# Swapping which engine copies which half of an expert's results, splitting the first chunk on two engines, and adding row sums with a reduction

## The chip, the cores and the metric

The kernel runs on one core of one Trainium2 chip. The core has a matrix engine (TensorE, in profiles PE, with its weight loads as PEld), a vector engine (VectorE, DVE), a scalar engine (ScalarE, ACT), a general engine (GpSimd, POOL) and a queue that issues transfers (SyncE, SP). Each works through its own list of instructions in order; they wait for each other through semaphores. The metric is the device time of one launch in microseconds. Three runs of the kernel before took 813.53, 816.81 and 817.45 us; the median is 816.81.

## The reference

Three layers follow each other: an attention in which a query sees only the keys of its own cluster, a mixture of eight experts with one expert for each token, and a layer with a rational activation. All is float32. Cut to what matters:

```python
# attention: 2 batches x 8 heads, 768 tokens, width 64, 16 clusters per head
mask = argmax(q_n @ c_n.T)[:, None] == argmax(k_n @ c_n.T)[None, :]
scores = where(mask, scale * q @ k.T, -1e9)
attn = exp(scores - rowmax)
attn = attn / (attn.sum(-1) + 1e-09)
x = attn @ v                                   # 1536 tokens x 512
# experts: 8, hidden width 1024, one expert per token
e, gate = argmax and its softmax weight of (xn @ en.T / tau)
x = gate * (maximum(x @ w1[e], 0) @ w2[e])
# last layer: hidden width 2048
h = x @ w_in
g = (a0 + a1*h + a2*h^2 + a3*h^3) / (1 + |b0|*|h| + |b1|*h^2 + 1e-6)
out = g @ w_out
```

## The kernel before, in words

Every float32 product is made of three products of rounded parts: a value is split into a high part (rounded to the format fp32r) and a low part (the value less the high part), and TensorE multiplies high by high, high by low and low by high (lines 489 to 491). So each operand needs a rounding copy and a subtraction, and these are spread over the engines.

**Attention.** Sixteen heads follow each other; a loop handles two heads a pass. A head has six row blocks (`i` = 0 to 5). For each block TensorE makes the scores, VectorE takes the row maximum (`rowmax`, NM, L953), ScalarE takes the exponential and its row sum (PR and SM, L624), TensorE transposes (L401), ScalarE makes the high part PTH (L651) and VectorE the low part PTL (L1040). TensorE's transposes of block `i` wait for the exponential of that block and for the two PTL halves of the block before. Beside this VectorE finds the clusters of the next head (`one_hots`, L963 to L971), and twice a head it turns three row sums into factors (`inverse_sums`, RS, L980 and L982): once behind block 4, and once behind block 1 of the next head. GpSimd splits the next head's operands (A, B) and values (VS, L855 and L857), and in heads 3 to 10 also one piece of the first expert's weights (`high_piece`, L825).

**Experts.** Tokens are sorted by expert and handled in chunks of 256 tokens; here each expert has one chunk, so there are eight. An expert has eight weight pieces of 128x1024 values: GpSimd rounds them (w_high, L825), VectorE subtracts (w_low, L1024). A chunk has a first product (four banks, rectified by ScalarE into HH, L734, and by VectorE into HL, L1171) and a second product into two banks, 6 and then 7. ScalarE copies bank 6 into YT rows 0 and 1 once the first half of the second product is done, while TensorE works on the second half; VectorE copies bank 7 into YT rows 2 and 3 at the end.

**The junction.** The last layer needs YT split into XH and XL. For the first chunk this is done by halves (`cut_first`): ScalarE rounds, VectorE subtracts. In between, ScalarE also rounds pieces 0 to 3 of w_out (L801). VectorE then makes w_low of pieces 4 to 7 of w_in. TensorE starts on the first half of three hidden pairs (`first_products`) when the first XL is there, and on the rest when the second is.

**The last layer.** Six chunks of eight hidden pairs. For a pair, ScalarE and VectorE evaluate the rational function in turns (VectorE lines 1220, 1222, 1224, 1231, 1233, 1235), ScalarE rounds it into HH (L759), GpSimd subtracts into HL (L901), and TensorE's second product of that pair, three pairs behind, waits for HL. In the first chunk VectorE makes w_low of one piece of w_out within each pair, between L1224 and L1231. GpSimd has to finish its rounding of w_out pieces 4 to 7 before its first HL.

The order on every engine is written out by hand; nothing is scheduled by a program.

Of the kernel before, what the change touches and what calls it, by code (L numbers as in the profile page):

```python
# [52 lines left out]
def program(nc, q, k, v, cent, emb, tau, w1, w2, w_in, w_out, coef_a, coef_b, cst, tokid, out, dbg=None):  # L53
# [4 lines left out]
    with ExitStack() as ctx:  # L58
# [64 lines left out]
        SM = esb("SM", [P, 2, JT])  # L123
# [49 lines left out]
        w_high, w_high_act, w_low = sem("w_high"), sem("w_high_act"), sem("w_low")  # L173
# [5 lines left out]
        yh_done, yl_done, g3_done, g4_done = (sem(n) for n in ("yh_done", "yl_done", "g3_done", "g4_done"))  # L179
# [31 lines left out]
        def _(sp):  # L211
# [44 lines left out]
            sp.wait_ge(pool_ready, 6)  # L256
# [64 lines left out]
        def _(pe):  # L321
# [268 lines left out]
        def _(act):  # L590
# [27 lines left out]
            def exp(g, par, i):  # L618
                n = JT * g + i
                act.wait_ge(max_done, n + 1)  # L620
                if needed(2 * n - 2):
# [3 lines left out]
                                     accum_out=SM[:, par, i:i + 1]).then_inc(exp_done, 1)  # L625
# [100 lines left out]
            with act.Fori(0, E // 2) as ep:  # L726
                for par in range(2):
                    lo, hi, off = bounds(act, 2 * ep + par)
                    with act.Fori(lo, hi) as i:
                        for fp in range(4):  # L730
                            if fp == 2:
# [7 lines left out]
                        act.wait_ge(y_ps, 2 * i + 1)  # L739
                        nc.scalar.activation(YT[:, 0:2, bass.ds(column(off, lo, i), CH)],  # L740
                                             PS[:, 6, :].rearrange("p (a t) -> p a t", a=2), ACT.Copy).then_inc(y_act, 1)
# [53 lines left out]
            total, = bounds(act, E - 1, (1,))  # L795
            act.wait_ge(y_act, total + 1)
            act.wait_ge(xl_done, total + 1)
# [16 lines left out]
        def _(pool):  # L814
# [5 lines left out]
            nc.gpsimd.memset(OH[:, :, :], 0.0).then_inc(pool_ready, 1)  # L820
            nc.gpsimd.memset(zeros[:, :], 0.0).then_inc(pool_ready, 1)
# [46 lines left out]
            pool.wait_ge(pool_ready, 6)  # L868
# [53 lines left out]
        def _(dve):  # L922
# [53 lines left out]
            def inverse_sums(g, par, grp):  # L976
# [3 lines left out]
                nc.vector.tensor_scalar(RS[:, :], SM[:, par, GT * grp:GT * (grp + 1)], 1e-9, None, ALU.add).then_inc(rs_done, 1)  # L980
# [233 lines left out]
            def layer_chunk(c, cpar, start=False, end=False):  # L1214
                for j in range(PAIRS):
# [9 lines left out]
                    if start:  # L1225
                        low_piece(E + 1, 1, j)
# [52 lines left out]
```

## Time and profile before

| what | value |
|---|---|
| median of three runs | 816.81 us |
| the profiled execution's own time | 815.08 us |
| its span, first to last instruction | 813.3 us |
| TensorE busy | 747.3 us, 92% of the span |
| VectorE busy | 607.1 us, 75% |
| ScalarE busy | 468.9 us, 58% |
| GpSimd busy | 350.1 us, 43% |
| mean granted TensorE clock | 0.969 of full speed |
| attention | about 0 to 300 us |
| routing of the tokens, TensorE nearly idle | about 300 to 329 us |
| experts | about 329 to 530 us |
| last layer | about 531 to 806 us |

The profile describes one execution. A row of the timeline has the start and the duration of one instruction (or of several alike, with their count), the engine, the line, the operation and, in brackets, how long the engine had been idle before and which instruction released it. The granted clock is the share of TensorE's full speed that the chip allowed in a stretch.

### The profile page before, as it was taken

The numbers are of one execution on the slowest core, as the hardware profiler recorded it, in microseconds if no ns is written. First come the engines' busy times: TensorE is split into PE (matmuls) and PEld (weight loads), VectorE is DVE, ScalarE is ACT, GpSimd is POOL, SyncE is SP. The second block draws the span as 40 slices with busy tenths as digits, with TensorE's granted clock in tenths as the row PEclk, the third lists the DMA queues.
The fourth block names the chain that finished last, engine by engine and source line by source line (L and its number), as shares of the span: only waits on it lengthen the run. The fifth ranks groups of instructions, "written<-read, shape, count | busy, mean of one in ns | idle before, by whom it ended". The sixth has DMA issues, their size and how long they took to land.

```text
span 813.3 us, 15460 instructions
## 1 busy us (share of the span) xinstructions
PE 747.3 (92%) x5289; PEld 695.2 (85%) x5290; DVE 607.1 (75%) x977; ACT 468.9 (58%) x884; POOL 350.1 (43%) x330
## 2 busy tenths in 40 slices
PE   7899999999999840699999999979999999999996
PEld 4799899998999730699999999979999999999995
DVE  4788888888888863356766666799987877877773
ACT  4677777778777850212222112457777767777672
POOL 3666757766566108204443344532232222322232
PEclk9999999999999985699999999999999999999999
DMA  9311112111110037224666444830000000000000
GB/s 266 85 32 31 39 29 48 29 29 39 29 58 1 0 107 278 63 97 175 225 235 232 158 170 169 286 104 1 1 27 1 26 3 1 26 0 26 0 26 27
DMA packets 67907, 64.66 MB, mean 80 GB/s; under 512 B 30872, under 2 KB 53528, under 8 KB 67872
## 3 DMA queue, kind: packets, MB, share of 16 engines
q1 hardware_dynamic: 65024, 57.29, 22.0%
q0 software_dynamic: 1920, 6.70, 2.1%
q8 instruction: 19, 0.31, 0.2%
q10 hardware_dynamic: 928, 0.23, 0.1%
q14 instruction: 16, 0.13, 0.0%
HBM read 56.92 MB, written 7.29 MB: 79 GB/s over the span
## 4 chain that ended last, share of the span: by engine, by line
PE 49%; issue 24%; DVE 13%; POOL 9%; ACT 3%; DMA 1%; POOLq 0%; DVEq 0%; ACTq 0%
PE PS L489 8%; PE PS L490 8%; PE PS L491 8%; PE PS L401 6%; POOL HL L901 6%; PE PS L375 3%; PE PS L376 3%; PE PS L360 3%; PE PS L361 3%; PE PS L342 3%; DVE NM L953 2%; DVE PTL L1040 2%; POOL xs_dram L892 2%; POOL out L910 1%; PE PS L384 1%
## 5 line engine op out<-in xcount | busy, mean ns | idle before, releaser
L489 PE MATMUL PS<-XH,w_high 128*128 128x256 f32 x640 | 182.9, 286 | 5.6 <-DVE XL L1163 2.5
L490 PE MATMUL PS<-XL,w_high 128*128 128x256 f32 x640 | 182.5, 285 | 0.0
L491 PE MATMUL PS<-XH,w_low 128*128 128x256 f32 x640 | 182.4, 285 | 0.0
L825 POOL TENSOR_SCALAR w_high<-w_raw 128x1024 fp32r<-128x1024 f32 x76 | 96.6, 1290 | 132.9 <-DMA w_raw<-in_moe_w 107.3
L901 POOL TENSOR_TENSOR HL<-U,HH 128x512 fp32r<-128x512 f32 x48 | 62.6, 1303 | 185.8 <-ACT HH L759 185.8
L489 PEld LDWEIGHTS PS<-XH,w_high 128*128 128x128 f32 x640 | 124.2, 194 | 8.6 <-issue 4.9
L490 PEld LDWEIGHTS PS<-XL,w_high 128*128 128x128 f32 x640 | 124.1, 194 | 1.8
L1040 DVE TENSOR_TENSOR PTL<-PS,PTH 128x384 fp32r<-128x384 f32 x192 | 97.9, 551 | 36.4 <-ACT PTH L651 36.3
L491 PEld LDWEIGHTS PS<-XH,w_low 128*128 128x128 f32 x640 | 124.0, 194 | 0.0
L1024 DVE TENSOR_TENSOR w_low<-w_raw,w_high 128x1024 fp32r<-128x1024 f32 x80 | 111.5, 1423 | 9.3 <-issue 9.2
L651 ACT ACTIVATE PTH<-PS 128x384 fp32r<-128x384 f32 x192 | 84.7, 489 | 45.3 <-PE PS L401 44.9
L953 DVE TENSOR_REDUCE NM<-PS 128x1 f32<-128x768 f32 x96 | 90.9, 948 | 2.6 <-PE PS L361 2.6
L401 PE MATMUL PS<-consts,PR 128*128 128x128 f32 x576 | 82.8, 278 | 9.8 <-ACT PR L624 5.1
L624 ACT ACTIVATE PR<-PS,NM 128x768 f32<-128x768 f32 x96 | 86.9, 905 | 5.5 <-DVE NM L953 5.3
L401 PEld LDWEIGHTS PS<-consts,PR 128*128 128x128 f32 x576 | 65.7, 143 | 19.2 <-DVE PTL L1040 7.9
L734 ACT ACTIVATE HH<-PS 128x512 fp32r<-128x512 f32 x32 | 19.1, 598 | 108.9 <-PE PS L491 108.9
L489 PE MATMUL PS<-w_high,HH 128*128 128x512 f32 x192 | 76.1, 396 | 2.8 <-POOL HL L901 2.8
L490 PE MATMUL PS<-w_low,HH 128*128 128x512 f32 x192 | 75.8, 395 | 0.0
L491 PE MATMUL PS<-w_high,HL 128*128 128x512 f32 x192 | 75.2, 392 | 0.0
L360 PE MATMUL PS<-B,A 128*128 128x512 f32 x192 | 73.3, 382 | 0.8 <-POOL A L866 0.8
L489 PE MATMUL PS<-HH,w_high 128*128 128x256 f32 x256 | 73.2, 286 | 0.0
L490 PE MATMUL PS<-HL,w_high 128*128 128x256 f32 x256 | 72.5, 283 | 0.0
(174 smaller groups left out, 1702.2 us busy)
## 6 DMA issues: line engine op xcount, KB each, us to landing
w_raw<-in_moe_w SPq DMA_DIRECT2D x64, 512.0 KB, 8.2
xs<-xs_dram SPq DMA_DIRECT2D x9, 578.0 KB, 7.7
w_raw<-in_moe_w_in SPq DMA_DIRECT2D x8, 512.0 KB, 8.2
w_raw<-in_moe_w_out SPq DMA_DIRECT2D x8, 512.0 KB, 6.3
QK<-in_q SPq DMA_DIRECT2D x16, 192.0 KB, 3.1
V<-in_v SPq DMA_DIRECT2D x16, 192.0 KB, 2.3
QK<-in_k SPq DMA_DIRECT2D x15, 192.0 KB, 3.2
xs_dram<-zeros SPq DMA_DIRECT2D x1, 578.0 KB, 3.3
```

The source lines that it names most:

```text
L360: nc.tensor.matmul(o[:, lo:hi], A1[par][:, cols], B1[par][:, lo:hi], start=True, stop=False)
L401: last = nc.tensor.transpose(pt_bank[hf][:, j * P:(j + 1) * P], PR[i % 2][:, c:c + P], ident)
L489: nc.tensor.matmul(o, wh, xh, start=first, stop=False)
L490: nc.tensor.matmul(o, wh, xl, start=False, stop=False)
L491: return nc.tensor.matmul(o, wl, xh, start=False, stop=last)
L624: nc.scalar.activation(PR[i % 2][:, :], s_bank(i % 2), ACT.Exp, bias=NM[:, par, i:i + 1], accum_out=SM[:, par, i:i + 1]).then_inc(exp_done, 1)
L651: nc.scalar.activation(PTH[grp][:, 3 * hf:3 * hf + 3, at:at + P], pt_bank[hf].rearrange("p (a q) -> p a q", a=3), ACT.Copy).then_inc(pth_d ...
L825: return nc.gpsimd.tensor_scalar(HIGH[par][:, p, :], RAW[par][:, p, :], 1.0, 0.0, ALU.mult, ALU.add)
L901: nc.gpsimd.tensor_tensor(HL[:, g:g + 2, :].rearrange("p a t -> p (a t)"), U[j % 2][:, :], HH[:, g:g + 2, :].rearrange("p a t -> p (a t)") ...
L953: nc.vector.tensor_reduce(NM[:, par, i:i + 1], s_bank(i % 2), AX.X, ALU.max, negate=True).then_inc(max_done, 1)
L1024: nc.vector.tensor_tensor(LOW[par][:, p, :], RAW[par][:, p, :], HIGH[par][:, p, :].bitcast(F32), ALU.subtract).then_inc(w_low, 1)
L1040: nc.vector.tensor_tensor(PTL[i // GT][:, 3 * hf:3 * hf + 3, at:at + P], pt_bank[hf].rearrange("p (a q) -> p a q", a=3), PTH[i // GT][:, 3 ...
```

## The change

Four edits.

1. **Row sums.** SM gets a second column next to each sum, filled once with 1e-9 by GpSimd. In `inverse_sums` VectorE adds each pair with `tensor_reduce`, where it added the constant 1e-9 with `tensor_scalar`.
2. **Expert results.** VectorE copies bank 6 (rows 0 and 1, after the first half of the second product); ScalarE copies bank 7 (rows 2 and 3, at the end).
3. **First chunk.** Rows 0 and 1 are rounded by VectorE itself (a `tensor_scalar`) and subtracted there; rows 2 and 3 are rounded by ScalarE. ScalarE no longer rounds pieces of w_out: GpSimd rounds all eight.
4. **First pair.** In the last layer's first pair, VectorE makes the low part of w_out piece 0 at the end of the pair and not in its middle.

```diff
-        SM = esb("SM", [P, 2, JT])
+        SM = esb("SM", [P, 2, JT, 2])
...
+            nc.gpsimd.memset(SM[:, :, :, 1:2], 1e-9).then_inc(pool_ready, 1)
...
-                nc.vector.tensor_scalar(RS[:, :], SM[:, par, GT * grp:GT * (grp + 1)], 1e-9, None, ALU.add).then_inc(rs_done, 1)
+                nc.vector.tensor_reduce(RS[:, :], SM[:, par, GT * grp:GT * (grp + 1), :], AX.X, ALU.add).then_inc(rs_done, 1)
...
-                        act.wait_ge(y_ps, 2 * i + 1)
-                        nc.scalar.activation(YT[:, 0:2, ...], PS[:, 6, :]..., ACT.Copy).then_inc(y_act, 1)
+                        act.wait_ge(y_ps, 2 * i + 2)
+                        nc.scalar.activation(YT[:, 2:4, ...], PS[:, 7, :]..., ACT.Copy).then_inc(y_act, 1)
...
-            act.wait_ge(y_act, total + 1)
             act.wait_ge(xl_done, total + 1)
-            cut_first(0)
-            for p in range(4):
-                act.wait_ge(raw_in[1][p // 2], 32 * (E // 2) + 32)
-                nc.scalar.activation(HIGH[1][:, p, :], RAW[1][:, p, :], ACT.Copy).then_inc(w_high_act, 1)
-            act.wait_ge(y_dve, total + 1)
+            act.wait_ge(y_act, total + 1)
             cut_first(1)
...
-                for p in range(4 if w == E + 1 else 0, 8):
+                for p in range(8):
                     high_piece(w, w % 2, p).then_inc(w_high, 1)
...
-                dve.wait_ge(y_ps, 2 * i + 2)
-                nc.vector.tensor_copy(YT[:, 2:4, ...], PS[:, 7, :]...).then_inc(y_dve, 1)
+                dve.wait_ge(y_ps, 2 * i + 1)
+                nc.vector.tensor_copy(YT[:, 0:2, ...], PS[:, 6, :]...).then_inc(y_dve, 1)
...
+                if n == 0:
+                    dve.wait_ge(y_dve, total + 1)
+                    dve.wait_ge(xl_done, total + 1)
+                    nc.vector.tensor_scalar(XH[0][:, 0:2, :], YT[:, 0:2, 0:CH], 1.0, 0.0, ALU.mult, ALU.add).then_inc(yh_done, 1)
...
-                    if start:
+                    if start and j:
                         low_piece(E + 1, 1, j)
...
+                    if start and j == 0:
+                        low_piece(E + 1, 1, 0)
```

The first place is on VectorE, in the loop over heads, behind block 1: before

```order
94 L969 TENSOR_REDUCE AM<-AEQ 128x12 [waits arg_step]
96 L971 TENSOR_TENSOR OH<-AEQ,AM 128x6x2x16 [waits arg_step]
98 L953 TENSOR_REDUCE NM<-PS 128x1 [waits s_done]
100 L980 TENSOR_SCALAR RS<-SM 128x3 [waits exp_done]
102 L982 RECIPROCAL RS<-RS 128x3 [waits rs_done]
```

and now:

```order
94 L965 TENSOR_REDUCE AM<-AEQ 128x12 [waits arg_step]
96 L967 TENSOR_TENSOR OH<-AEQ,AM 128x6x2x16 [waits arg_step]
98 L949 TENSOR_REDUCE NM<-PS 128x1 [waits s_done]
100 L976 TENSOR_REDUCE RS<-SM 128x3 [waits exp_done]
102 L978 RECIPROCAL RS<-RS 128x3 [waits rs_done]
```

Nothing moved here; one instruction has another kind, and keeps its wait.

The second place is on VectorE at the junction, from the split of the first chunk to the end of the last layer's first pair. Before:

```order
407 L1203 TENSOR_TENSOR XL<-YT,XH 128x512 [waits yh_done] x2
408 L1024 TENSOR_TENSOR w_low<-w_raw,w_high 128x1024 [waits w_high] x4
409 L1220 TENSOR_TENSOR PS<-PS,AH 128x512 [waits t_done]
410 L1222 TENSOR_TENSOR U<-U,PS 128x512
411 L1224 SCALAR_TENSOR_TENSOR U<-U,minus_a,PS 128x512 [waits v_done]
412 L1024 TENSOR_TENSOR w_low<-w_raw,w_high 128x1024 [waits w_high_act]
413 L1231 SCALAR_TENSOR_TENSOR PS<-PS,R 128x512 [waits r0_done]
414 L1233 SCALAR_TENSOR_TENSOR R<-PS,R 128x512 [waits n_done]
415 L1235 SCALAR_TENSOR_TENSOR U<-U,minus_a,R 128x512 [waits r_done]
416 L1220 TENSOR_TENSOR PS<-PS,AH 128x512 [waits t_done]
```

and now:

```order
409 L1199 TENSOR_SCALAR XH<-YT 128x512 [waits xl_done,y_dve]
410 L1203 TENSOR_TENSOR XL<-YT,XH 128x512 [waits yh_done]
411 L1203 TENSOR_TENSOR XL<-YT,XH 128x512 [waits yh_act]
412 L1017 TENSOR_TENSOR w_low<-w_raw,w_high 128x1024 [waits w_high] x4
413 L1220 TENSOR_TENSOR PS<-PS,AH 128x512 [waits t_done]
414 L1222 TENSOR_TENSOR U<-U,PS 128x512
415 L1224 SCALAR_TENSOR_TENSOR U<-U,minus_a,PS 128x512 [waits v_done]
416 L1231 SCALAR_TENSOR_TENSOR PS<-PS,R 128x512 [waits r0_done]
417 L1233 SCALAR_TENSOR_TENSOR R<-PS,R 128x512 [waits n_done]
418 L1235 SCALAR_TENSOR_TENSOR U<-U,minus_a,R 128x512 [waits r_done]
419 L1017 TENSOR_TENSOR w_low<-w_raw,w_high 128x1024 [waits w_high]
420 L1220 TENSOR_TENSOR PS<-PS,AH 128x512 [waits t_done]
```

VectorE gets one rounding more, and the low part of the first w_out piece stands behind the first pair's last step.

The third place is on GpSimd, from the end of w_in's pieces to the first HL. Before:

```order
210 L825 TENSOR_SCALAR w_high<-w_raw 128x1024 [waits raw_in0_2] x2
211 L825 TENSOR_SCALAR w_high<-w_raw 128x1024 [waits raw_in0_3] x2
212 L825 TENSOR_SCALAR w_high<-w_raw 128x1024 [waits raw_in1_2] x2
213 L825 TENSOR_SCALAR w_high<-w_raw 128x1024 [waits raw_in1_3] x2
214 L901 TENSOR_TENSOR HL<-U,HH 128x512 [waits gh_done] x8
```

and now:

```order
211 L821 TENSOR_SCALAR w_high<-w_raw 128x1024 [waits raw_in0_2] x2
212 L821 TENSOR_SCALAR w_high<-w_raw 128x1024 [waits raw_in0_3] x2
213 L821 TENSOR_SCALAR w_high<-w_raw 128x1024 [waits raw_in1_0] x2
214 L821 TENSOR_SCALAR w_high<-w_raw 128x1024 [waits raw_in1_1] x2
215 L821 TENSOR_SCALAR w_high<-w_raw 128x1024 [waits raw_in1_2] x2
216 L821 TENSOR_SCALAR w_high<-w_raw 128x1024 [waits raw_in1_3] x2
217 L897 TENSOR_TENSOR HL<-U,HH 128x512 [waits gh_done] x8
```

Four roundings stand ahead of the four that were there.

## Rows read from the trace of the kernel before

**Rows 1.** Busy time by stage, loop over heads: engines' busy us (instructions), clock, DMA.
```profile
60.00:250.00 190.00, 186.05 (x1359) 173.25 (x1357) 163.86 (x329) 147.46 (x327) 127.18 (x133) 1.00 0.14 36
```

**Rows 2.** TensorE's waits: for whom, us in total, times, longest.
```profile
PE PS L401 <- DVE PTL L1040: 4.7, 13, 0.4
```

**Rows 3.** Line 980 over the span: ns least/median/most.
```profile
L980 DVE TENSOR_SCALAR RS<-SM x32: 155/159/772, 38.2 to 292.9; 128x3 f32<-128x3 f32 x32
```

**Rows 4.** Timeline of VectorE, blocks 0 and 1: start, us, instruction.
```profile
63.40 0.36 DVE L971 TENSOR_TENSOR OH<-AEQ,AM 128x192 bf16<-128x192 f32 x1
63.68 0.95 DVE L953 TENSOR_REDUCE NM<-PS 128x1 f32<-128x768 f32 x1
64.55 0.70 DVE L980 TENSOR_SCALAR RS<-SM 128x3 f32<-128x3 f32 x1
...
65.40 1.02 DVE L1040 TENSOR_TENSOR PTL<-PS,PTH 128x384 fp32r<-128x384 f32 x2
...
266.38 0.70 DVE L980 TENSOR_SCALAR RS<-SM 128x3 f32<-128x3 f32 x1
```

**Rows 5.** Timeline of GpSimd, the same stretch.
```profile
63.40 0.73 POOL L855 TENSOR_SCALAR VS<-V 128x384 fp32r<-128x384 f32 x1 [1.02 <-PE PS L376]
64.21 1.01 POOL L857 TENSOR_TENSOR VS<-V,VS 128x384 fp32r<-128x384 f32 x1
```

**Rows 6.** Timeline of ScalarE, the same: end of block 2's exponential.
```profile
65.55 0.19 ACT L624 ACTIVATION_READ_ACCUMULATOR PR<-PS,NM 128x1 f32 x1
```

**Rows 7.** Timeline of TensorE, the transposes of blocks 2 and 3.
```profile
66.02 1.01 PE L401 MATMUL PS<-consts,PR 128*128 128x128 f32 x6 [0.37 <-DVE PTL L1040]
66.79 0.48 PE L360 MATMUL PS<-B,A 128*128 128x512 f32 x1
...
68.96 0.81 PE L401 MATMUL PS<-consts,PR 128*128 128x128 f32 x6
69.53 0.48 PE L360 MATMUL PS<-B,A 128*128 128x512 f32 x1
```

**Rows 8.** Timeline of VectorE and GpSimd, first head.
```profile
27.19 0.35 DVE L969 TENSOR_REDUCE AM<-AEQ 128x12 f32<-128x192 f32 x1
27.58 1.48 DVE L971 TENSOR_TENSOR OH<-AEQ,AM 128x192 bf16<-128x192 f32 x1
...
27.02 1.82 POOL L845 TENSOR_TENSOR B<-T,B 64x768 fp32r<-64x768 f32 x1
```

**Rows 9.** Timeline of VectorE and ScalarE, between experts 6 and 7.
```profile
505.94 0.69 DVE L1179 COPY YT<-PS 128x512 f32 x1 [3.26 <-PE PS L491]
...
508.56 0.60 ACT L734 ACTIVATE HH<-PS 128x512 fp32r<-128x512 f32 x1 [7.84 <-PE PS L491]
```

**Rows 10.** Timeline of VectorE, junction.
```profile
530.44 1.47 DVE L1203 TENSOR_TENSOR XL<-YT,XH 128x512 fp32r<-128x512 f32 x2
...
537.76 0.70 DVE L1220 TENSOR_TENSOR PS<-PS,AH 128x512 f32<-128x512 f32 x1 [0.46 <-ACT PS L785]
...
539.75 1.22 DVE L1024 TENSOR_TENSOR w_low<-w_raw,w_high 128x1024 fp32r<-128x1024 f32 x1
...
542.34 1.09 DVE L1235 SCALAR_TENSOR_TENSOR U<-U,minus_a,R 128x512 f32<-128x512 f32 x1
```

**Rows 11.** Timeline of GpSimd, junction.
```profile
534.72 3.50 POOL L825 TENSOR_SCALAR w_high<-w_raw 128x1024 fp32r<-128x1024 f32 x2 [10.35 <-DMA w_raw<-in_moe_w_out]
539.82 3.07 POOL L825 TENSOR_SCALAR w_high<-w_raw 128x1024 fp32r<-128x1024 f32 x2 [1.60 <-DMA w_raw<-in_moe_w_out]
544.17 1.28 POOL L901 TENSOR_TENSOR HL<-U,HH 128x512 fp32r<-128x512 f32 x1 [1.28 <-ACT HH L759]
```

**Rows 12.** Timeline of TensorE, junction.
```profile
531.18 0.39 PE L489 MATMUL PS<-XH,w_high 128*128 128x256 f32 x1 [1.64 <-DVE XL L1203]
...
545.50 0.51 PE L489 MATMUL PS<-w_high,HH 128*128 128x512 f32 x1 [2.56 <-POOL HL L901]
```

**Rows 13.** Busy time and granted clock behind the junction.
```profile
546.00:552.00 6.00, 6.00 (x30) 5.20 (x29) 5.89 (x9) 4.52 (x8) 1.28 (x1) 0.72 0.01 3
```

More of the change, by code:

```diff
@@ L172, in program @@
         raw_in = [[sem(f"raw_in{n}_{i}") for i in range(4)] for n in range(2)]
-        w_high, w_high_act, w_low = sem("w_high"), sem("w_high_act"), sem("w_low")
+        w_high, w_low = sem("w_high"), sem("w_low")
         tau_in, xs_scaled = sem("tau_in"), sem("xs_scaled")
@@ L178, in program @@
         hh_done, hl_done, y_ps, y_act, y_dve = (sem(n) for n in ("hh_done", "hl_done", "y_ps", "y_act", "y_dve"))
-        yh_done, yl_done, g3_done, g4_done = (sem(n) for n in ("yh_done", "yl_done", "g3_done", "g4_done"))
+        yh_done, yh_act, yl_done, g3_done, g4_done = (sem(n) for n in ("yh_done", "yh_act", "yl_done", "g3_done", "g4_done"))
         ah_done, u_done, t_done, root_done, r0_done = (sem(n) for n in ("ah_done", "u_done", "t_done", "root_done", "r0_done"))
@@ L795, in _ @@
             total, = bounds(act, E - 1, (1,))
+            act.wait_ge(xl_done, total + 1)
             act.wait_ge(y_act, total + 1)
-            act.wait_ge(xl_done, total + 1)
-            cut_first(0)
-            for p in range(4):
-                act.wait_ge(raw_in[1][p // 2], 32 * (E // 2) + 32)
-                nc.scalar.activation(HIGH[1][:, p, :], RAW[1][:, p, :], ACT.Copy).then_inc(w_high_act, 1)
-            act.wait_ge(y_dve, total + 1)
             cut_first(1)
@@ L1019, in low_piece @@
             def low_piece(w, par, p):
-                if isinstance(w, int) and w == E + 1:
-                    dve.wait_ge((w_high_act, w_high)[p // 4], (p + 1, 8 * w + p - 3)[p // 4])
-                else:
-                    dve.wait_ge(w_high, 8 * w + p + 1)
+                dve.wait_ge(w_high, 8 * w + p + 1)
                 nc.vector.tensor_tensor(LOW[par][:, p, :], RAW[par][:, p, :], HIGH[par][:, p, :].bitcast(F32), ALU.subtract).then_inc(w_low, 1)
@@ L1177, in chunk @@
                         low_piece(e + 1, 1 - par, p)
-                dve.wait_ge(y_ps, 2 * i + 2)
-                nc.vector.tensor_copy(YT[:, 2:4, bass.ds(column(off, lo, i), CH)],
-                                      PS[:, 7, :].rearrange("p (a t) -> p a t", a=2)).then_inc(y_dve, 1)
+                dve.wait_ge(y_ps, 2 * i + 1)
+                nc.vector.tensor_copy(YT[:, 0:2, bass.ds(column(off, lo, i), CH)],
+                                      PS[:, 6, :].rearrange("p (a t) -> p a t", a=2)).then_inc(y_dve, 1)
             dve.drain().then_inc(y_dve, 1)
@@ L1200, in cut_first @@
             def cut_first(n):
-                dve.wait_ge(yh_done, n + 1)
+                if n == 0:
+                    total, = bounds(dve, E - 1, (1,))
+                    dve.wait_ge(y_dve, total + 1)
+                    dve.wait_ge(xl_done, total + 1)
+                    nc.vector.tensor_scalar(XH[0][:, 0:2, :], YT[:, 0:2, 0:CH], 1.0, 0.0, ALU.mult, ALU.add).then_inc(yh_done, 1)
+                    dve.wait_ge(yh_done, 1)
+                else:
+                    dve.wait_ge(yh_act, 1)
                 nc.vector.tensor_tensor(XL[0][:, 2 * n:2 * n + 2, :], YT[:, 2 * n:2 * n + 2, 0:CH], XH[0][:, 2 * n:2 * n + 2, :].bitcast(F32),
```

18 lines of the change are left out of this document (9 added, 9 removed).

## The prediction

> **What bounds the kernel now.** I read the busy time by stage first. In the loop over heads TensorE is busy for 186.05 of 190 us at full clock [rows 1]: it is the bound, and only its gaps can be won. TensorE's list of waits says whose they are: 13 times it waits for VectorE's PTL, 4.7 us in total, never over 0.4 us [rows 2]. These are one wait per head. I followed it back on VectorE's timeline, and there stands a suspicious row: the addition of a constant to three numbers takes 0.70 us [rows 4]. Over the span that instruction takes 155 ns at least, 159 ns in the median and 772 ns at most [rows 3]; on the timeline it is long 14 times, each time behind block 1, the last at 266.38 us [rows 4], and short behind block 4.
>
> Why it is long is seen on GpSimd: its VS subtraction runs from 64.21 to 65.22 us [rows 5], and the small addition, which started at 64.55, ends at 65.25 [rows 4]. VectorE did not compute for 0.70 us; it was held until GpSimd's instruction was over, and the PTL that TensorE needs starts at 65.40 behind it.
>
> At the junction of experts and last layer TensorE waits 1.64 us for the first XL and 2.56 us for the first HL [rows 12], and behind that the granted clock is 0.72 for 6 us [rows 13].
>
> **The change part by part.** *Row sums.* 14 held instructions lose their hold if the reduction is not held. In the first head a `tensor_reduce` from SBUF took 0.35 us beside a running GpSimd subtraction (27.02 to 28.84 us), while the `tensor_tensor` with two SBUF inputs right behind it took 1.48 us and ended when GpSimd had (29.06) [rows 8]. So reductions pass. The new one reads 6 elements for a partition where that one read 192; it costs between 0 and 0.35 us. I take 0.16, the median of the old one [rows 3], since both are tiny. VectorE then gains 0.70 - 0.16 = 0.54 us a head.
>
> The Trainium skill ("SBUF — State Buffer", practical consequences of the port rules) says that `copy`, `cast` and `tensor_scalar` can take the port pair shared with GpSimd, that it is an exclusive lock, and that `tensor_reduce` on trn2 never contends. The held `tensor_scalar` and the reduction that passed agree with it.
>
> How much of 0.54 reaches TensorE? PTL would start at 64.86, and its first half, 0.51 us (half of 1.02), be there at 65.4, the second at 65.9 [rows 4]. TensorE is free at 66.02 - 0.37 = 65.65 [rows 7]. But its transposes of block 2 also need block 2's exponential, and ScalarE ends that at 65.55 + 0.19 = 65.74 [rows 6]; it hangs on the row maximum at 63.68, ahead of the saved time. So TensorE starts at about 65.80 and not 66.02: 0.22 us. Next, the transposes of block 2 take 66.79 - 66.02 = 0.77 us to the next product, where those of block 3 take 69.53 - 68.96 = 0.57 us [rows 7]; the second three wait for the second PTL half. That one is now in time: 0.20 us more. Together 0.42 us a head. What is late next is the exponential, by 0.15 us. Heads: 13, by the waits [rows 2]; at the fourteenth, in the last pair of heads, ScalarE has extra squares to do and holds TensorE, so I count nothing. 13 x 0.42 = 5.5 us. The lower end is 13 x 0.22 = 2.9, the upper 13 x (0.37 + 0.20) = 7.4 us.
>
> *The fill of SM with 1e-9* is one small fill on GpSimd at the start. VectorE and GpSimd wait for it, but long before they have inputs: nothing. If that cover were gone it would be some 0.1 to 0.2 us once.
>
> *The swap of the result copies.* Both are off TensorE's path. In the middle of the second product VectorE now has the 0.7 us copy, and at the end ScalarE. ScalarE's last copy ends near 506.6, where VectorE's does now, and its first rectification comes at 508.56, after 7.84 us of idleness [rows 9]: 1.9 us are left for the loop's register loads. If these took longer, HH and HL would be late, but TensorE needs HL only after all four banks of the first product. Nothing, eight times. Behind ScalarE's wait only that rectification is queued.
>
> *The first chunk's split.* XH and XL of rows 0 and 1 can be made while TensorE works on the second half of the last expert, where before the XL waited behind VectorE's final copy. If nothing holds VectorE, the wait of 1.64 us [rows 12] goes. But VectorE's next steps do not come sooner: the second XL still ends at about 531.9 [rows 10] and the four w_low pieces behind it near 537.3, so the first pair's chain starts at 537.3 and not 537.76, 0.46 us earlier [rows 10]. TensorE's early start is given back at its next wait, the first HL.
>
> *GpSimd's four extra roundings.* GpSimd is idle for 10.35 us before 534.72 [rows 11], and 4 pieces at 1.5 us (half of 3.07) take 6 us. They fit into the gap, if their data is there, which ScalarE used without a wait.
>
> *The moved w_low piece* takes 1.22 us out of the first pair's chain [rows 10], about 1.1 without the overlap at its start. The first HH could come 0.46 + 1.1 = 1.6 us earlier. GpSimd however ends its last pieces at 542.89 and makes HL from 544.17 [rows 11]: at most 1.28 us can be won. Against that, w_low now stands where HL wants to start, and the last step L1235 took 1.09 us with GpSimd active [rows 10]. If HL is held for the rest of one w_low, some 0.8 us go. And the second pair's chain hardly starts earlier, as VectorE's total work is the same. The clock will drop again behind the wait: nothing won there.
>
> Junction in all: 1.3 us won at best; 0.5 lost at worst short of a rival below, if VectorE's new rounding and both XL are each held by one of GpSimd's new pieces. I take 0.5 us won, near the middle. VectorE's rounding of 128x512 has no row; it lies between 0.16 [rows 3] and 0.69, the copy of that size [rows 9], and I use 0.5; it is hidden unless held.
>
> By the same page of the Trainium skill this step speaks against the change: the new rounding is a `tensor_scalar` and the subtractions have two SBUF inputs, so each can be blocked by GpSimd's four new pieces. By that rule alone the junction would win 0.4 us and not 1.3.
>
> **Sum.** 5.5 + 0.5 = 6.0 us. The profiled execution took 815.08 us, so 809.1 on its own terms. It lies 1.73 us below the median of 816.81; the mean of the three runs is 815.9. I predict 815.9 - 6.0 = 810.
>
> **Rivals.** *Saved but given back:* the exponential, or GpSimd's masks of the next head, sets the pace as soon as PTL is earlier, and the second wait stays. Then 2.9 us and nothing at the junction: 813. For it: only 0.15 us lie between the old bound and the next. Against it: blocks 3 to 5 have idle engines before them.
>
> *No effect:* the reduction is held too, or the long row has another cause. Only the junction's 0.5 remains: 815.4. Against it stand rows 8, for it only that they show one case.
>
> *A new hold, slower:* in each head VectorE's OH starts at 63.40, in the same moment as GpSimd's VS rounding [rows 4, 5], and it has two SBUF inputs. When it comes second it is held, as in the first head: 1.48 instead of 0.36 us, 1.12 more [rows 4, 8]. The row maximum, the exponential and TensorE's transposes would follow: start at 65.80 + 1.12 = 66.92 and not 66.02, less 0.20 for the second half: 0.7 us a head, 13 x 0.7 = 9.1 us, so about 824 with the junction at -0.5. It decides once OH comes after GpSimd's start. Against it: both starts hang on TensorE's work of that block, which the change doesn't shift against them, and in the heads of the loop OH was never held.
>
> *More:* the full 7.4 us in attention, 1.3 at the junction, and the clock, 6 us at 0.72, so 6 x 0.28 = 1.7 us, stays up [rows 13]: 815.9 - 10.4 = 805.5. Against it: the first HL stays a wait of over 2 us.
>
> **How the numbers follow.** A difference of 0.5% of the median, 4.1 us, is about what a measurement can tell from no change; faster means under 812.7, slower over 820.9. Forecast 0.70, own range 806.5 to 813.5, of which 0.60 is faster and 0.10 same. Given back 0.11: 0.04 faster, 0.07 same. No effect 0.06, same 0.05 and slower 0.01. Slower rival 0.05. More 0.08, all faster. Faster 0.72, same 0.22, slower 0.06. The range runs from 804.5 to 814.5.
>
> **What would show it.** Right: all 32 row sums at about 0.16 us; TensorE's waits for PTL gone or replaced by about 0.15 us for ScalarE's PR; one head (201.83 us for the 12 from 64.55 to 266.38, so 16.82 us) shorter by 0.42 us; at the junction the first TensorE wait under 1.1 us, a second one of over 2 us, and the clock low behind it. Wrong: a row sum of 0.7 us; OH at over 1 us; a head as long as before; TensorE waiting in the experts for YT, HH or HL.

## The result, and the profile after

| kernel | median of 7 runs | from - to | ratio to before |
|---|---|---|---|
| before | 816.08 us | 813.53 - 817.45 | |
| changed | 812.65 us | 810.43 - 813.88 | 0.9959, 95% interval 0.9941 to 0.9977 |

The change gains 3.4 us (1.9 to 4.8 by the interval), where 6.0 were forecast. The profiled execution of the changed kernel took 812.02 us, its span is 810.1 us and its mean clock 0.968; before it was 815.08, 813.3 and 0.969. Line numbers have shifted: RS is L976 (was L980), PTL L1033 (L1040), NM L949 (L953), HL L897 (L901), w_low L1017 (L1024), w_high L821 (L825).

First the row sums, over the whole span (it answers to [rows 3]):

```profile
L976 DVE TENSOR_REDUCE RS<-SM x32: 146/148/158, 38.3 to 289.3; 128x3 f32<-128x6 f32 x32
```

The longest of 32 now takes 158 ns; the hold is gone. Fourteen of them still start while GpSimd's VS subtraction runs, and take 0.15 us each; in the kernel before the 14 in that place were the long ones. TensorE's waits for the PTL halves, against [rows 2], and the loop over heads, against [rows 1]:

```profile
PE PS L401 <- ACT PR L624: 5.4, 8, 1.4
PE PS L401 <- DVE PTL L1033: 2.5, 12, 0.2
```

```profile
60.00:250.00 190.00, 187.47 (x1378) 176.15 (x1378) 161.16 (x336) 149.88 (x334) 129.10 (x136) 1.00 0.14 36
```

The waits are shorter but still there, 0.2 us each. TensorE is busy for 1.4 us more of the same 190. The timeline of the stretch of [rows 4 to 7], VectorE and GpSimd first, then ScalarE, then TensorE:

```profile
63.12 0.36 DVE L967 TENSOR_TENSOR OH<-AEQ,AM 128x192 bf16<-128x192 f32 x1
63.40 0.95 DVE L949 TENSOR_REDUCE NM<-PS 128x1 f32<-128x768 f32 x1
64.27 0.15 DVE L976 TENSOR_REDUCE RS<-SM 128x3 f32<-128x6 f32 x1
64.45 0.18 DVE L978 RECIPROCAL RS<-RS 128x3 f32<-128x3 f32 x1
64.57 1.02 DVE L1033 TENSOR_TENSOR PTL<-PS,PTH 128x384 fp32r<-128x384 f32 x2
```

```profile
63.12 0.73 POOL L851 TENSOR_SCALAR VS<-V 128x384 fp32r<-128x384 f32 x1 [1.00 <-PE PS L376]
63.93 1.00 POOL L853 TENSOR_TENSOR VS<-V,VS 128x384 fp32r<-128x384 f32 x1
```

```profile
65.27 0.19 ACT L624 ACTIVATION_READ_ACCUMULATOR PR<-PS,NM 128x1 f32 x1
```

```profile
65.60 0.87 PE L401 MATMUL PS<-consts,PR 128*128 128x128 f32 x6 [0.22 <-DVE PTL L1033]
66.22 0.48 PE L360 MATMUL PS<-B,A 128*128 128x512 f32 x1
```

The reduction starts inside GpSimd's subtraction (63.93 to 64.93) and ends inside it. PTL starts 1.17 us after NM's start and not 1.72. OH, which the slower rival feared for, still begins together with GpSimd's VS and takes 0.36 us. TensorE's gap went from 0.37 to 0.22 us, and the stretch from the transposes to the next product from 0.77 to 0.62. A head, by this row and the one of the same place eleven heads later, takes (247.55 - 65.60) / 11 = 16.54 us, where it took 16.82:

```profile
247.55 0.87 PE L401 MATMUL PS<-consts,PR 128*128 128x128 f32 x6 [0.21 <-DVE PTL L1033]
```

At the junction, VectorE (answers to [rows 10]), GpSimd [rows 11] and TensorE [rows 12]:

```profile
523.75 0.68 DVE L1172 COPY YT<-PS 128x512 f32 x1
524.46 0.56 DVE L1199 TENSOR_SCALAR XH<-YT 128x512 fp32r<-128x512 f32 x1
525.05 1.40 DVE L1203 TENSOR_TENSOR XL<-YT,XH 128x512 fp32r<-128x512 f32 x1
527.57 0.69 DVE L1203 TENSOR_TENSOR XL<-YT,XH 128x512 fp32r<-128x512 f32 x1 [1.11 <-ACT XH L752]
528.18 4.62 DVE L1017 TENSOR_TENSOR w_low<-w_raw,w_high 128x1024 fp32r<-128x1024 f32 x4
533.09 0.70 DVE L1220 TENSOR_TENSOR PS<-PS,AH 128x512 f32<-128x512 f32 x1 [0.29 <-ACT PS L785]
```

```profile
534.97 2.06 POOL L821 TENSOR_SCALAR w_high<-w_raw 128x1024 fp32r<-128x1024 f32 x2 [0.23 <-DMA w_raw<-in_moe_w_out]
538.31 1.51 POOL L897 TENSOR_TENSOR HL<-U,HH 128x512 fp32r<-128x512 f32 x1 [1.29 <-ACT HH L759]
```

```profile
526.51 0.39 PE L489 MATMUL PS<-XH,w_high 128*128 128x256 f32 x1 [0.58 <-DVE XL L1203]
...
539.88 0.50 PE L489 MATMUL PS<-w_high,HH 128*128 128x512 f32 x1 [1.60 <-POOL HL L897]
...
582.37 0.39 PE L491 MATMUL PS<-w_high,HL 128*128 128x512 f32 x1
...
587.63 0.47 PE L489 MATMUL PS<-w_high,HH 128*128 128x512 f32 x1 [2.00 <-ACT OUT L766]
```

The wait for the first XL fell from 1.64 to 0.58 us and the wait for the first HL from 2.56 to 1.60. The last row is new: TensorE wants to start on the second chunk's second product, whose banks still hold the first chunk's results, and waits 2.00 us until ScalarE has copied them (OUT, L766, at 586.91). The row ahead of it is the first chunk's last matmul into those banks: they were complete about 4 us before the copy began. No such wait was listed before. The granted clock moved with the waits: behind the first HL, against [rows 13], it is now 1.00, and the 0.72 stands behind the OUT wait:

```profile
540.00:546.00 6.00, 5.78 (x36) 5.07 (x36) 5.90 (x9) 4.49 (x9) 1.29 (x1) 1.00 0.01 3
...
586.00:592.00 6.00, 4.37 (x12) 3.50 (x13) 5.81 (x11) 5.21 (x9) 2.39 (x2) 0.72 0.01 3
```

### The profile page after: what moved, and what is told of

It is laid out like the page before. It is cut to its first block, busy times and chain, and to the rows that moved or that the text cites. A ratio compares the mean times of both kernels' runs of the same rounds, so it can differ in the third digit from the quotient of the medians.

```text
span 810.1 us, 15464 instructions
## 1 busy us (share of the span) xinstructions
PE 745.9 (92%) x5289; PEld 695.7 (86%) x5290; DVE 596.8 (74%) x978; ACT 463.4 (57%) x879; POOL 354.6 (44%) x335
## 4 chain that ended last, share of the span: by engine, by line
PE 47%; issue 25%; DVE 13%; POOL 9%; ACT 3%; DMA 1%; DVEq 0%; POOLq 0%; ACTq 0%
PE PS L489 8%; PE PS L491 7%; PE PS L490 7%; PE PS L401 6%; POOL HL L897 6%; PE PS L375 3%; PE PS L376 3%; PE PS L360 3%; PE PS L361 3%; PE PS L342 3%; DVE NM L949 2%; DVE PTL L1033 2%; DVE w_low L1017 2%; POOL xs_dram L888 2%; POOL out L906 1%
## 5 line engine op out<-in xcount | busy, mean ns | idle before, releaser
L821 POOL TENSOR_SCALAR w_high<-w_raw 128x1024 fp32r<-128x1024 f32 x80 | 100.6, 1277 | 126.6 <-DMA w_raw<-in_moe_w 107.2
L897 POOL TENSOR_TENSOR HL<-U,HH 128x512 fp32r<-128x512 f32 x48 | 62.7, 1307 | 188.4 <-ACT HH L759 188.4
L1033 DVE TENSOR_TENSOR PTL<-PS,PTH 128x384 fp32r<-128x384 f32 x192 | 98.0, 552 | 40.1 <-ACT PTH L651 40.0
L1017 DVE TENSOR_TENSOR w_low<-w_raw,w_high 128x1024 fp32r<-128x1024 f32 x80 | 108.6, 1387 | 0.9 <-issue 0.9
L949 DVE TENSOR_REDUCE NM<-PS 128x1 f32<-128x768 f32 x96 | 90.9, 948 | 2.6 <-PE PS L361 2.6
L401 PE MATMUL PS<-consts,PR 128*128 128x128 f32 x576 | 81.0, 277 | 8.0 <-ACT PR L624 5.4
L491 PE MATMUL PS<-HH,w_low 128*128 128x256 f32 x256 | 72.5, 283 | 0.0
```

Of the source, the lines that this page charges most:

```text
L401: last = nc.tensor.transpose(pt_bank[hf][:, j * P:(j + 1) * P], PR[i % 2][:, c:c + P], ident)
L491: return nc.tensor.matmul(o, wl, xh, start=False, stop=last)
L821: return nc.gpsimd.tensor_scalar(HIGH[par][:, p, :], RAW[par][:, p, :], 1.0, 0.0, ALU.mult, ALU.add)
L897: nc.gpsimd.tensor_tensor(HL[:, g:g + 2, :].rearrange("p a t -> p (a t)"), U[j % 2][:, :], HH[:, g:g + 2, :].rearrange("p a t -> p (a t)") ...
L949: nc.vector.tensor_reduce(NM[:, par, i:i + 1], s_bank(i % 2), AX.X, ALU.max, negate=True).then_inc(max_done, 1)
L1017: nc.vector.tensor_tensor(LOW[par][:, p, :], RAW[par][:, p, :], HIGH[par][:, p, :].bitcast(F32), ALU.subtract).then_inc(w_low, 1)
```

## How the segments are compared

Runs of one kernel spread over some 3 to 4 us, as much as the gain. Much of that goes with the granted clock: of the 40 runs of the kernel before that stood beside the experiments, the eight with a mean clock of 0.964 took 815.8 to 818.0 us, the six with 0.970 to 0.972 took 813.4 to 815.4. The profiles show where part of that lies: block 2 of the fourth head starts at 63.38 us in E9's profile and at 65.67 in E10's, though their attention is the same. So I compare segments of TensorE's timeline: the first transposes of the experts (L485), the first product with XH, the first with HL, the end of the span. One point of ScalarE's is added, the start of its first copy of OUT, since it will be needed. Each ratio further down is against runs of the kernel before that were taken with that experiment: their medians are 816.35 us for E1 to E4, 815.46 for E5 to E8 and 815.82 for E9 and E10.

| kernel | experts start | first XL [wait] | first HL [wait] | end | start to first XL | first XL to end | first XL to OUT copy |
|---|---|---|---|---|---|---|---|
| before | 329.10 | 531.18 [1.64] | 545.50 [2.56] | 813.3 | 202.1 | 282.1 | 60.45 |
| changed | 325.40 | 526.51 [0.58] | 539.88 [1.60] | 810.1 | 201.1 | 283.6 | 60.40 |
| E1 | 326.28 | 528.40 [1.64] | 542.96 [2.77] | 810.7 | 202.1 | 282.3 | 60.69 |
| E2 | 329.84 | 529.85 [0.59] | 543.26 [1.62] | 811.9 | 200.0 | 282.1 | 60.45 |
| E3 | 329.48 | 530.13 [0.59] | 543.52 [1.61] | 812.2 | 200.7 | 282.1 | 60.43 |
| E4 | 323.54 | 524.14 [0.58] | 537.54 [1.63] | 806.2 | 200.6 | 282.1 | 60.47 |
| E5 | 325.97 | 525.97 [0.60] | 540.58 [2.83] | 808.4 | 200.0 | 282.4 | 60.77 |
| E6 | 325.57 | 527.58 [1.64] | 541.28 [1.92] | 810.0 | 202.0 | 282.4 | 60.74 |
| E7 | 327.50 | 528.73 [0.60] | 541.97 [1.47] | 810.5 | 201.2 | 281.8 | 59.84 |
| E8 | 325.86 | 526.90 [0.67] | 540.15 [1.47] | 807.6 | 201.0 | 280.7 | 59.05 |
| E9 | 324.38 | 525.62 [0.60] | 538.89 [1.50] | 806.2 | 201.2 | 280.6 | 59.03 |
| E10 | 324.94 | 527.34 [1.64] | 541.38 [2.27] | 807.9 | 202.4 | 280.6 | 58.94 |

## Which edit brings the gain: E1 and E2

E1 is the kernel before with edit 1 alone (and the column of 1e-9 that it needs):

```diff
-                nc.vector.tensor_scalar(RS[:, :], SM[:, par, GT * grp:GT * (grp + 1)], 1e-9, None, ALU.add).then_inc(rs_done, 1)
+                nc.vector.tensor_reduce(RS[:, :], SM[:, par, GT * grp:GT * (grp + 1), :], AX.X, ALU.add).then_inc(rs_done, 1)
```

> The kernel before with the row sums alone changed (pairs added by the reduction). Theory: the attention gives all that the row sums can, 13 heads at about 0.28 us, so the experts' first transposes start at about 325.4 us and the whole is about 3.6 us shorter than before; the junction is as before (waits of 1.64 and 2.56 us, low clock behind the second). Rival: the shorter attention is given back or enlarged at the junction; then the difference to before is under 2 or over 5 us.

E2 is the changed kernel with the same edit the other way round, so with edits 2 to 4 alone.

> The changed kernel with the row sums as before. Theory: attention as before (transposes at about 329.1 us); the junction wins some 1.9 us at the first HL, but VectorE cannot follow, TensorE waits about 2 us for ScalarE's OUT copy in the second chunk and the clock drops behind it, so the whole is within 0.5 us of before. Rival: the three other edits have a value of their own, then it is 1.5 us or more below before; or they cost, then it is above.

Measured: E1 812.70 us (6 runs), ratio 0.995 (0.993 to 0.997), E2 815.70 us (12 runs), ratio 0.9996 (0.998 to 1.0011), beside 816.35 for the kernel before. The row sums alone bring all that can be measured; edits 2 to 4 alone bring, by E2's interval, at most 0.2% of 816, or 1.6 us. E2's row sums have their long form back, and TensorE's waits for PTL with them:

```profile
L975 DVE TENSOR_SCALAR RS<-SM x32: 150/159/774, 38.7 to 293.5; 128x3 f32<-128x3 f32 x32
```

```profile
PE PS L401 <- DVE PTL L1032: 4.2, 12, 0.4
```

## Why the old row sum was long: E3

E3 is the changed kernel with the same column of 1e-9, but added by an operation with two SBUF inputs:

```diff
-                nc.vector.tensor_reduce(RS[:, :], SM[:, par, GT * grp:GT * (grp + 1), :], AX.X, ALU.add)
+                nc.vector.tensor_tensor(RS[:, :], SM[:, par, GT * grp:GT * (grp + 1), 0], SM[:, par, GT * grp:GT * (grp + 1), 1], ALU.add)
```

> The changed kernel with the two columns of SM added by a tensor_tensor, two inputs from SBUF, in place of the reduction. Theory (GpSimd's subtraction holds every VectorE instruction that takes a second SBUF port): the sums behind block 1 take about 0.7 us again, those behind block 4 about 0.16, and the span is 3 to 4 us longer than that of the changed kernel. Rival (only the tensor_scalar form is slow, or its constant): all sums take about 0.16 us and the span is that of the changed kernel, 810 us.

One run: 814.11 us, span 812.2. The span is 2.1 us longer than the changed kernel's and not 3 to 4 as expected; the experts start 4.1 us later (329.48 against 325.40), and the changed kernel's profile loses 1.6 us again behind the junction, as shown below. The hold is back, in the same place and to the same end. VectorE's row, GpSimd's beside it, and the operation over the span:

```profile
64.86 0.69 DVE L976 TENSOR_TENSOR RS<-SM 128x3 f32<-128x3 f32 x1
```

```profile
64.53 1.00 POOL L853 TENSOR_TENSOR VS<-V,VS 128x384 fp32r<-128x384 f32 x1
```

```profile
L976 DVE TENSOR_TENSOR RS<-SM x32: 150/153/694, 38.5 to 293.0; 128x3 f32<-128x3 f32 x32
```

The row sum ends at 65.55, GpSimd at 65.53. All 14 row sums behind block 1 are long in this way, 0.69 us each, and end 0.01 to 0.02 us behind the subtraction. TensorE waits 13 times for PTL, 4.4 us in total. So it isn't the second column or its fill that takes the hold away, but the kind of operation. The Trainium skill ("SBUF — State Buffer", section "Who interferes with whom") states that `tensor_reduce` never contends for the port pair that VectorE shares with GpSimd, that `tensor_scalar` can and that `tensor_tensor` with both inputs in SBUF does. The three kinds that stood in this one place agree: `tensor_scalar` 0.70, `tensor_tensor` 0.69, `tensor_reduce` 0.15 us.

## Why 0.27 us a head and not 0.42: E4

In the changed kernel the exponential of block 2 ends at 65.27 + 0.19 = 65.46, and the first PTL half near 65.08 (half of 1.02 behind 64.57). Both are there at 65.46, yet TensorE starts at 65.60. The profile names PTL as releaser, though that was done 0.5 us before. In the loop over heads TensorE's queue holds a wait of its own for the exponential, and the matrix product behind it waits for PTL: two waits one after the other. E4 is the changed kernel with the waits in the other order:

```diff
-                        pe.wait_ge(exp_done, n + 1)
                         for hf in range(2):
                             if needed(2 * n - 1 + hf):
                                 pe.wait_ge(ptl_done, 2 * n - 1 + hf)
+                            if hf == 0:
+                                pe.wait_ge(exp_done, n + 1)
```

> The changed kernel with TensorE's two waits ahead of a block's transposes in the other order: PTL first, the exponential second. Theory: what is left of the gap at block 2 is the exponential plus 0.1 us in which TensorE's queue works out the second wait after the first is over; the gap falls from 0.21 to about 0.1 us, 13 x 0.1 = 1.3 us less, transposes of the experts at about 324.1 us. Rival: the gap ends with the second half of PTL (65.59 us, TensorE at 65.60); then it stays 0.21 us and nothing changes.

Measured: 811.76 us (6 runs), ratio 0.9943 (0.9923 to 0.9962). ScalarE and TensorE in the same block:

```profile
63.92 0.19 ACT L625 ACTIVATION_READ_ACCUMULATOR PR<-PS,NM 128x1 f32 x1
```

```profile
64.17 0.87 PE L402 MATMUL PS<-consts,PR 128*128 128x128 f32 x6 [0.20 <-ACT PR L625]
```

The exponential ends at 64.11, TensorE starts 0.06 us later and not 0.14, and the releaser named is the exponential. The rival, that the second PTL half releases TensorE, falls: VectorE's PTL row is 63.22 to 64.24 here, and TensorE starts at 64.17. But the gap itself is 0.20 us where it was 0.22, and about 0.1 was expected. A head takes 16.47 us (64.17 to 245.34, 11 heads) where it took 16.54. That is 0.07 x 13 = 0.9 us, as the medians have it (812.65 - 811.76), though their intervals overlap. So the exponential is what bounds this place now. By the head's length the order of the two waits is worth 0.07 us, a third of the gap; how a gap that is only 0.02 us shorter goes with it isn't settled.

## What the junction's edits do: E5 and E6

E5 is the changed kernel with w_low of w_out's piece 0 back in the middle of the first pair (edit 4 undone):

```diff
-                    if start and j:
+                    if start:
                         low_piece(E + 1, 1, j)
...
-                    if start and j == 0:
-                        low_piece(E + 1, 1, 0)
```

> The changed kernel with the low part of w_out piece 0 back in the middle of the first pair. Theory: the first HL comes 1.1 us later against the end of the experts than in the changed kernel, so TensorE waits about 2.7 us there and not 1.6, and the waits behind it (0.24 us at the next HL, 2.0 us at the OUT copy) shrink by as much in sum; the whole stays within 1 us of the changed kernel. Rival: the early first HL is what the other edits bring at the junction; then the whole is 1 to 2 us longer.

E6 is the kernel before with edits 1 and 4: E1 with the first of these lines the other way round.

> The kernel before with the new row sums and the moved low part alone; the results' copies, the first chunk's split and the rounding of w_out as before. Theory: the first HL waits for GpSimd or for the first pair's chain; it comes about 1.1 us earlier than with the row sums alone, where TensorE waited 2.77 us for it, so the wait is about 1.6 us; TensorE is then ahead of VectorE less than in the changed kernel, by the 0.5 us that the split gave, and waits about 1 us for the OUT copy. Whole: within 1 us of the changed kernel. Rival: without the early split the moved low part brings nothing, the wait stays at 2.6 us or more.

Measured: E5 812.49 us (5 runs), ratio 0.9953 (0.9935 to 0.9971); E6 811.92 us (4 runs), ratio 0.9948 (0.9928 to 0.9968). In the times neither stands apart from the changed kernel, as both theories had it. In the traces edit 4 does its part: with it the wait for the first HL is 1.60 and 1.92 us, without it 2.83 and 2.77 (changed and E6 against E5 and E1 in the table). Edit 3 takes 1.0 us from the wait for the first XL, in all eight kernels that have it. But from the first XL to the end E1, E5 and E6 need 282.3 to 282.4 us, the kernel before 282.1 and the changed one 283.6. Where the first HL comes late, no OUT wait is listed; where it comes early, OUT is waited for. In E6 it was expected at about 1 us and is 1.98. E6, TensorE:

```profile
541.28 0.50 PE L489 MATMUL PS<-w_high,HH 128*128 128x512 f32 x1 [1.92 <-POOL HL L902]
```

```profile
PE PS L489 <- ACT OUT L766: 2.0, 1, 2.0
```

The table's last column shows what this place hangs on. From the first XL to the start of ScalarE's copy of OUT it is 60.4 to 60.8 us in the kernel before, the changed one and E1 to E6, wherever w_low stands, however long HL was waited for, and whether the clock behind it was low (before, E1, E5) or not. The matmul behind it starts 0.72 us after the start of that copy in the kernel before too, where no wait is listed. Before, ScalarE and TensorE, then ScalarE in the changed kernel, whose matmul is at 587.63:

```profile
591.63 0.58 ACT L766 ACTIVATE OUT<-PS 128x512 f32<-128x512 f32 x1
```

```profile
592.35 0.47 PE L489 MATMUL PS<-w_high,HH 128*128 128x512 f32 x1
```

```profile
586.91 0.58 ACT L766 ACTIVATE OUT<-PS 128x512 f32<-128x512 f32 x1
```

From that copy to the end all of these need 221.6 to 221.7 us. Only the changed kernel needs 223.2, with the low clock behind its OUT wait.

In the first chunk of the last layer VectorE has its six steps for each pair and eight pieces of w_low. In the changed kernel its timeline lists no idle time from 533.09 to 594 us. It and ScalarE come to the copies of OUT only in the middle of the second chunk's third pair, behind all of this. What TensorE gains ahead of that, it waits for there.

## Taking the work from VectorE, or moving the copy: E7 and E8

E7 gives w_low of w_out's pieces 4 to 7 to GpSimd, one behind each of its first four HL:

```diff
             for j in range(PAIRS):
                 low(j, j)
+                if j < 4:
+                    pool.wait_ge(w_high, 8 * (E + 1) + j + 5)
+                    nc.gpsimd.tensor_tensor(LOW[1][:, j + 4, :], RAW[1][:, j + 4, :], HIGH[1][:, j + 4, :].bitcast(F32), ALU.subtract).then_inc(w_low_pool, 1)
```

> The changed kernel with GpSimd making the low parts of w_out pieces 4 to 7, in its idle time of the first chunk. Theory: VectorE is the bound of the first chunk (no idle time from 528 to 594 us), so 4 x 1.14 us less work there lets it keep up with TensorE: the wait of 2.0 us for the OUT copy goes, and with it the low clock that the profile shows behind it, 2 to 3.7 us less than the changed kernel. Rival: GpSimd's longer instructions hold VectorE's two-input ones and delay HL; then new waits for HL of over 1 us appear and the gain is under 1 us.

E8 leaves the work where it is, and moves the copies of the results forward in the third pair: on VectorE from behind L1224 to behind the pair's first product, on ScalarE from behind the inverse root to ahead of it.

```diff
                     dve.wait_ge(t_done, s + 1)
                     nc.vector.tensor_tensor(den, den, AH[:, :], ALU.mult).then_inc(q_done, 1)
+                    if j == LAG - 1 and not start:
+                        results(c - 1)
...
-                    if j == LAG - 1 and not start:
-                        results(c - 1)
-
                     dve.wait_ge(r0_done, s + 1)
```

> The changed kernel with the OUT copies of both engines moved forward within the third pair of a chunk (ScalarE ahead of the inverse root, VectorE behind the first product). Theory: the wait of 2.0 us for the OUT copy is one of order as much as of work: TensorE has the chunk's results ready some 4 us before ScalarE takes them; moved forward the wait falls to under 0.7 us, 1.3 us less, or up to 3 where the clock fell behind it. Rival: VectorE's total work in the first chunk sets the pace; the wait moves to the next HL and the gain is under 0.5 us.

Measured: E7 812.33 us (6 runs), ratio 0.9945 (0.9927 to 0.9962); E8 809.59 us (6 runs), ratio 0.9922 (0.9906 to 0.9939). In E7 the OUT wait is gone, but GpSimd needs 2.40 and then 3.40 us for a piece that VectorE makes in 1.2, and the second HL is late behind it:

```profile
540.41 1.51 POOL L899 TENSOR_TENSOR HL<-U,HH 128x512 fp32r<-128x512 f32 x1 [1.40 <-ACT HH L761]
541.88 2.40 POOL L914 TENSOR_TENSOR w_low<-w_raw,w_high 128x1024 fp32r<-128x1024 f32 x1
548.23 1.27 POOL L899 TENSOR_TENSOR HL<-U,HH 128x512 fp32r<-128x512 f32 x1 [3.95 <-ACT HH L761]
549.47 3.40 POOL L914 TENSOR_TENSOR w_low<-w_raw,w_high 128x1024 fp32r<-128x1024 f32 x1
```

```profile
549.56 0.50 PE L489 MATMUL PS<-w_high,HH 128*128 128x512 f32 x1 [1.66 <-POOL HL L899]
```

In E8 the OUT wait falls from 2.00 to 0.76 us, and the clock behind it is 1.00:

```profile
586.67 0.47 PE L489 MATMUL PS<-w_high,HH 128*128 128x512 f32 x1 [0.76 <-ACT OUT L766]
```

```profile
586.00:592.00 6.00, 5.33 (x33) 4.85 (x34) 5.90 (x9) 4.62 (x9) 1.62 (x2) 1.00 0.01 3
```

From the first XL to the end it takes 280.7 us, 1.4 less than before, and all of that lies ahead of the OUT copy (59.05 against 60.45 us from the first XL). So the copy's place in VectorE's and ScalarE's order sets the pace here. Whether the junction's gain now passes as well is not shown by E8; E10 below has the order without the junction. ScalarE in E8:

```profile
585.95 0.58 ACT L766 ACTIVATE OUT<-PS 128x512 f32<-128x512 f32 x1
```

## Both improvements, and without the junction: E9 and E10

E9 is E8 with E4's order of waits. E10 is E9 without edits 2 to 4: the kernel before with the row sums by reduction, E4's order and E8's moved copies.

> The changed kernel with both improvements at once: the result copies of the first chunk moved forward in the third pair, and TensorE's transposes waiting for PTL before the exponential. Theory: the two act in different stages, so the gains add. TensorE's wait for the copied results stays at about 0.8 us, the first-HL wait at about 1.5 us, a head of the loop is about 16.47 us (against 16.54), and the time is 809.59 - 11 x 0.07 = 808.8 us, ratio about 0.991. Rival: what the wait order seemed to give is only the spread between executions; then head 16.54 and 809.6 us.

> The kernel before with the row sums by reduction, PTL waited for before the exponential, and the result copies moved forward: everything of the best version but the change's edits 2 to 4. Theory: edits 2 to 4 are worth something only once the wait for the copied results is gone. Then this one has a first-XL wait of 1.64 us and a first-HL wait of about 2.8 us with the low clock behind it, the time from the first XL to the end is about 282.3 us less nothing (the 2.0 us wait for the copies is not there in that kernel), and it is slower than the best version by about 1.0 us at the first XL and 1.2 to 1.7 us behind it: 811 us. Rival: edits 2 to 4 are worth nothing here either, as VectorE's total work in the first chunk is the same: within 0.5 us of the best version, and the time from the first XL wait to the end like its 280.7 us.

Measured, side by side: E9 810.21 us (808.15 to 811.67, 6 runs), ratio 0.9927 (0.991 to 0.9943); E10 809.67 us (808.83 to 812.46, 6 runs), ratio 0.9926 (0.9909 to 0.9943). In both a head takes 16.47 us. Neither time can be told from E8's, where E9 was expected 0.8 us below it, so the wait order isn't proven by times; its rows stand. And E10 is as fast as E9. Here my theory was wrong and the rival right: E10 waits 2.27 us for the first HL, but then only 0.40 for OUT, and from the first XL to the end both need 280.6 us. Its copy of OUT starts 58.94 us behind the first XL, E9's 59.03. The moved copy brings its 1.4 us with or without the junction's edits, and a longer wait for HL ahead of it costs nothing. E10, TensorE:

```profile
527.34 0.39 PE L490 MATMUL PS<-XH,w_high 128*128 128x256 f32 x1 [1.64 <-DVE XL L1205]
541.38 0.50 PE L490 MATMUL PS<-w_high,HH 128*128 128x512 f32 x1 [2.27 <-POOL HL L903]
...
587.01 0.47 PE L490 MATMUL PS<-w_high,HH 128*128 128x512 f32 x1 [0.40 <-ACT OUT L767]
```

What is left of edits 2 to 4 is the 1.0 us at the first XL, which the profiles of E9 and E10 show (201.2 against 202.4 us from the experts' start) and their medians don't. Whether it reaches the time stays open. The medians of E8, E9 and E10 are 2.4 to 3.1 us below that of the changed kernel.

## Why the prediction was right, and where not

The forecast was 810.0 us with a range of 804.5 to 814.5; 812.65 lies in it. The likeliest outcome was to be faster by over 4.1 us, with a chance of 0.72; 3.4 us fall short of that. Direction and cause were right, and the size was overestimated: the main term, the heads, gave 3.6 of 5.5 us, and the junction nothing that the times show. That the measured time still lies in the range is owed to the range's width.

- *The old row sum is held by GpSimd, and a reduction passes.* Right: 32 row sums of 146 to 158 ns, 0.15 us where 0.16 was taken, and E3 shows it is the kind of operation.
- *0.42 us a head.* This is the term that was mis-sized: 16.82 - 16.54 = 0.28 us, and 0.27 to 0.28 times 13 is 3.6 us and not 5.5. It had two parts. The start of the transposes should come 0.22 us earlier, 0.06 behind the end of the exponential; it came 0.15 earlier, 0.14 behind. The second PTL half should give back 0.20; the stretch went from 0.77 to 0.62, not 0.57. The first is the second wait in TensorE's queue, of which E4 gives back 0.07. I had taken the latency between the exponential and TensorE as 0.06 us from no row. Why 0.62 and not 0.57 remains isn't settled.
- *That the exponential is late next.* Right, though the profile hid it under PTL's name until E4.
- *Swap of the result copies: nothing.* Right as far as seen: no wait of TensorE inside the experts for YT, HH or HL. No run undid the swap alone.
- *The junction: 0.5 us won, at best 1.3.* The pieces were larger than forecast. Counted from the start of the experts, the first pair's chain starts 0.97 us earlier (forecast 0.46), and TensorE gets the first HL 1.92 us earlier. The bound of 1.28 failed because it took the end of GpSimd's last pieces as fixed. Counted from the experts' start these ended 2.2 us earlier too: their data was there 1.15 us sooner, and they took 2.06 us where [rows 11] have 3.07. The first XL took 1.40 us where the next takes 0.69; GpSimd's roundings run from 517.13 to 527.36 without a gap beside it, so this is the feared hold. The rounding ahead of it took 0.56 us (0.5 was assumed) and wasn't held. The prediction's 0.4 us for a junction with such holds, and its 0.5 us lost at worst, have no sum behind them. But the sum failed at a step that was not in it: what TensorE gains at the first HL it waits for at the OUT copies 45 us later. The prediction said that VectorE's total work is the same and drew this conclusion for the second pair only, not for the last thing that TensorE wants from that chunk.
- *The clock stays low behind the first HL.* Wrong in place: it was low behind OUT. The 6 x 0.28 = 1.7 us cost differently there. Behind the first HL they lie ahead of the OUT copy, whose time they don't move (60.45 us from the first XL in the kernel before and in E2, with the low clock and without); behind the OUT wait they reach the end (223.2 against 221.6 us). So the 1.7 us of the rival "more" were not there to be won. In this execution that makes the junction with what follows 0.5 us slower than before, counted from the experts' start (484.7 against 484.2 us).
- *The rivals.* "Saved but given back" named the right kind of event for attention (the exponential sets the pace) and for the junction, and its 813 is nearer to 812.65 than my 810; but its claim that the second part of the head's gain stays away was wrong, since 0.15 of 0.20 us came. "No effect" fell by the row sums. The slower rival didn't occur: OH took 0.36 us. "More" fell by the same two bounds.

## What to carry to other kernels

A tiny instruction with an odd duration is worth a look at what GpSimd does at that moment: if it ends when GpSimd's instruction ends, another kind of operation with the same result may be free. Before adding up a saving per iteration, put down what is late next, and with what latency the waiting engine starts behind it; two waits in a row in a queue put the blame on the second. And where one engine is saturated for a whole stage, follow a gain to the last thing that stage delivers, since there it comes due: a wait that gets shorter ahead of it is worth only what it moves that delivery.

## What the runs showed of the hardware that was not expected

- A copy of 128x2 integers is held like the rest. In E8 VectorE's copy, which ends at 587.42, stands beside GpSimd's HL, which ends at 587.40, where the same copy took 0.16 us in the changed kernel. In six chunks its durations are 159 to 1006 ns; the five long ones each end 0.02 us behind an HL, and the short one has no GpSimd instruction beside it. So E8 pays up to 0.85 us of VectorE's time in a chunk for its new order. Whether avoiding that would shorten the whole was not run.

```profile
586.41 1.01 DVE L1212 COPY tok_now<-tok_sorted 128x2 int32 x1
```

```profile
586.12 1.28 POOL L897 TENSOR_TENSOR HL<-U,HH 128x512 fp32r<-128x512 f32 x1 [2.94 <-ACT HH L759]
```

- The granted clock at the waits. TensorE was idle for 2.56, 2.77 and 2.83 us ahead of the first HL in before, E1 and E5, and each time the clock behind was 0.72 over 6 us, so part of that stretch was at 1.2 GHz and the rest at 2.4. Behind all waits of 1.60 to 1.92 us for HL, and behind E10's 2.27, it was 1.00, which is 2.4 GHz. Behind the OUT wait it was 0.72 in the changed kernel (2.00 us) and 1.00 in E2, E3, E4 and E6 (2.01, 2.00, 2.03 and 1.98 us). Equal waits, then, need not have an equal clock behind them, and a single profile can charge to a change 1.6 us that are not in other executions of the same stretch. How often the changed kernel's executions have it, one profile doesn't tell.
